# Attention inputs loaded as 48 rows of each half, in two DMAs, with r and v in one buffer

## The reference, cut to what matters

```python
for t in range(S):
    y[:, :, t] = np.einsum('bhd,bhde->bhe', rt, state)
    Sa = np.einsum('bhde,bhe->bhd', state, at)
    state_decay = state * wt[:, :, None, :] - np.einsum('bhd,bhe->bhde', Sa, bt)
    state = state_decay + np.einsum('bhd,bhe->bhde', vt, kt)
```

## Time and profile before

| | |
|---|---|
| Time, median of 3 runs | 1083.21 us (1082.46 to 1086.68) |
| Span of the profiled execution | 1081.6 us (its own device time is not listed; 1.6 us below the median) |
| Busy: TensorE matmul, VectorE, ScalarE, GpSimd | 974.9, 605.9, 316.1, 285.7 us |
| Moved | 159.61 MB in 119,984 packets, mean 148 GB/s |
| `t_in` loads | 48 of 776 KB |
| `rr`, `vt`, `vtm` loads | 24 each of 384, 256 and 240 KB |

### The profile page before, as it was taken

The page is one execution under the profiler, slowest core; times in us unless marked ns, Lnnn a source line. Parts: engine busy times, 40 slices in busy tenths (PEclk is TensorE's granted clock), DMA queues, the critical chain, the costliest instruction groups (busy, mean ns, idle before and its releaser), DMA issues. The chain is left out here.

```text
span 1081.6 us, 47466 instructions
## 1 busy us (share of the span) xinstructions
PE 974.9 (90%) x21177; PEld 853.5 (79%) x21178; DVE 605.9 (56%) x981; ACT 316.1 (29%) x737; POOL 285.7 (26%) x351
## 2 busy tenths in 40 slices
PE   3425879999999998999999999979999999999997
PEld 3425769889888866888878888848999999999997
DVE  8896957898988761111211111146656565655655
ACT  5434645655555500011010010031121222222211
POOL 1008989798910003116611100051101000000000
PEclk9999977999999989999999999999999999999999
DMA  6877656998888537996884544320010101010100
GB/s 230 227 176 213 212 162 196 248 262 254 255 248 260 159 116 252 318 307 216 249 274 160 163 160 162 117 79 25 25 25 25 25 1 25 1 25 2 25 1 25
DMA packets 119984, 159.61 MB, mean 148 GB/s; under 512 B 60164, under 2 KB 91028, under 8 KB 119540
## 3 DMA queue, kind: packets, MB, share of 16 engines
q1 hardware_dynamic: 105636, 125.12, 38.5%
q0 software_dynamic: 5824, 25.28, 7.8%
q10 hardware_dynamic: 8464, 8.43, 2.4%
HBM read 133.15 MB, written 19.23 MB: 141 GB/s over the span
## 5 line engine op out<-in xcount | busy, mean ns | idle before, releaser
L1102 DVE TENSOR_SCALAR ht<-h_bank 128x512 f32<-128x512 f32 x62 | 42.8, 691 | 233.4 <-PE h_bank L1079 233.3
L1365 ACT CAST g_hi<-g 128x512 fp32r<-128x512 f32 x96 | 59.6, 620 | 278.6 <-DVE g L1319 278.6
L1090 PE MATMUL y_bank<-w_all,ht 128*128 x496 | 140.4, 437 | 0.3 <-DVE ht L1102 0.3
L1090 PEld LDWEIGHTS y_bank<-w_all,ht 128*128 128x128 f32 x496 | 92.7, 192 | 35.6 <-issue 1.9
L1234 PE MATMUL y_bank<-w_out_hi,g_hi 128*128 128x320 f32 x380 | 118.0, 311 | 1.4 <-DVE g_lo L1299 1.4
L1079 PE MATMUL h_bank<-xt,w 128*128 128x128 f32 x992 | 119.0, 278 | 0.0
L1234 PE MATMUL y_bank<-w_out_hi,g_lo 128*128 128x320 f32 x380 | 117.5, 309 | 0.0
L1234 PE MATMUL y_bank<-w_out_lo,g_hi 128*128 128x320 f32 x380 | 117.3, 309 | 0.0
L1079 PEld LDWEIGHTS h_bank<-xt,w 128*128 128x128 f32 x992 | 113.1, 192 | 3.8
L1221 PE MATMUL h_bank<-xt_hi,w_in_hi 128*128 128x512 f32 x288 | 113.8, 395 | 0.5 <-DVE xt_hi L1282 0.5
L1221 PE MATMUL h_bank<-xt_hi,w_in_lo 128*128 128x512 f32 x288 | 112.6, 391 | 0.0
(11 more groups left out here) (207 smaller groups left out, 1763.4 us busy)
## 6 DMA issues: line engine op xcount, KB each, us to landing
w<-w_in SPq DMA_DIRECT2D x31, 1024.0 KB, 5.9
t_in<-wab_in SPq DMA_DIRECT2D x24, 776.0 KB, 6.2
t_in<-wak_in SPq DMA_DIRECT2D x24, 776.0 KB, 6.7
w_all<-w_in POOLq DMA_DIRECT2D x8, 1280.0 KB, 8.9
rr<-rr_in SPq DMA_DIRECT2D x24, 384.0 KB, 3.3
w_rest<-w_in SPq DMA_DIRECT2D x62, 128.0 KB, 3.1
vt<-vt_in SPq DMA_DIRECT2D x24, 256.0 KB, 3.9
vtm<-vtm_in SPq DMA_DIRECT2D x24, 240.0 KB, 3.4
```

The lines of the kernel that those rows point to most:

```text
L1090: last = pe.matmul(y_bank[s][:, 0:FEAT], ht[s][:, f, :], w2[:, ds(e * W2 + f * FEAT, FEAT)], start=f == 0, stop=f == NF - 1)
L1102: dve.tensor_scalar(ht[s][:, FH * n:FH * n + FH, :].rearrange("q f t -> q (f t)"), h_bank[s][n][:, :], 0.0, None, ALU.max).then_inc(s_relu, 1)
L1365: act.copy(g_hi[j % RING][:, :], g[j % 2][:, :]).then_inc(s_ghi, 1)
```

## The change

Three things are changed. A `t_in` load is issued as two DMAs, one for each half; from the fourth load on each brings 48 rows of the half in place of 64 (`filled`), and VectorE waits for 32 in place of 16. The first three loads still bring all 64 rows, so that the rows not loaded later hold the padding of an earlier load. `rr` and `vt` become parts of one buffer `vr` with 20 blocks of 64 columns, loaded as 48 rows of each half in two DMAs, where `rr` was loaded and with its wait for `m2`. `load_vt`, with its wait for `m1`, is gone.

```diff
+FILLED = 48
+
+
+def filled(i):
+    return slice(HALF * i, HALF * i + FILLED)
...
-        g2, m1, m2, sat, vt = (m_.sb(n, [PARTS, HS, C]) for n in ("g2", "m1", "m2", "sat", "vt"))
-        rr = m_.sb("rr", [PARTS, HS + HP, C])
+        g2, m1, m2, sat = (m_.sb(n, [PARTS, HS, C]) for n in ("g2", "m1", "m2", "sat"))
+        vr = m_.sb("vr", [PARTS, 2 * HS + HP, C])
+        rr, vt = vr[:, 0:HS + HP, :], vr[:, HS + HP:2 * HS + HP, :]
...
-                sp.dma_start(t_in[j % TR][:, :], src).then_inc(s_t[j % TR], 16)
+                for h in two:
+                    part = rows(h) if j < TR else filled(h)
+                    sp.dma_start(t_in[j % TR][part, :], src[part, :]).then_inc(s_t[j % TR], 16)
...
-            def load_rr(k):
+            def load_vr(k):
                 if k >= 1:
                     sp.wait_ge(did["m2"], k)
-                sp.dma_start(rr[:, :, :], inp["rr"][k]).then_inc(s_vt_rr, 16)
+                for h in two:
+                    sp.dma_start(vr[filled(h), :, :], inp["vr"][k][filled(h)]).then_inc(s_vr, 16)
...
-            def load_vt(k):
-                if k >= 1:
-                    sp.wait_ge(did["m1"], k)
-                sp.dma_start(vt[:, :, :], inp["vt"][k]).then_inc(s_vt_rr, 16)
...
                 if k == 21:
-                    load_rr(0)
+                    load_vr(0)
...
                 if k == STEPS - 2:
                     load_vtm(0)
-                    load_vt(0)
...
                 if more:
                     load_vtm(k + 1)
-                    load_vt(k + 1)
                 if k + 2 < STEPS:
                     load_inverses(k + 2)
                 if more:
-                    load_rr(k + 1)
+                    load_vr(k + 1)
...
-                dve.wait_ge(s_t[j % TR], 16 * (j // TR + 1))
+                dve.wait_ge(s_t[j % TR], 32 * (j // TR + 1))
...
-                arrive(s_vt_rr, 32 * i)
+                arrive(s_vr, 32 * i)
...
-    arrays["vt"] = halves(by_head(v))
-    arrays["rr"] = halves(np.concatenate([by_head(r), other_half(by_head(r))], axis=3))
+    arrays["vr"] = halves(np.concatenate([by_head(r), other_half(by_head(r)), by_head(v)], axis=3))
```

More of the change, by code:

```diff
@@ L234, in attention @@
         s_blk, s_tt = ([[m_.sem(f"{n}{s}_{part}") for part in range(GROUP)] for s in range(3)] for n in ("s_blk", "s_tt"))
-        s_ax_vtm, s_vt_rr = (m_.sem(n) for n in ("s_ax_vtm", "s_vt_rr"))
+        s_ax_vtm, s_vr = (m_.sem(n) for n in ("s_ax_vtm", "s_vr"))
         s_step, s_step_dve = m_.sem("s_step"), m_.sem("s_step_dve")
```

## The result

The change takes 1094.04 us (median of 20 runs, 1084.99 to 1102.83) against 1083.18 us for the kernel before in the same session (20 runs, 1077.10 to 1088.55). The ratio is 1.0093, with a 95% interval of 1.0070 to 1.0115: slower by 0.9%. The forecast was 1078.2 us, with a chance of 0.08 for slower, so it had the wrong sign. The profiled execution of the change took 1094.93 us with a span of 1093.1 us; the span before was 1081.6 us.

What follows compares the result with a forecast made beforehand. Bounds: VectorE's waits for `t_in` behind a late queue in the first stage, TensorE in the second. Savings 2.1 + 1.2 + 0.8 + 1.0 - 0.1 = 5.0 us gave 1078.2 us; forecast's own range 1075 to 1082, overall 1070 to 1084.

Steps and rivals of the forecast that it cites:

- the first of the sum: Bytes of the attention loads: a `t_in` load takes 0.48 us less transfer time, `rr` and `vt` as `vr` 0.40 less.
- Waits at 39 to 48 us, 2.1 us less: First stage: most of VectorE's 2.36 us of waits for `t_in` go; 2.1 us taken, bounds 1.0 to 2.36.
- at 81 and 87 us, 1.2 less: First stage, after the inversion by halves: VectorE's 2.34 us of `t_in` waits shrink by 1.2 us, bounds 0 to 2.34.
- the sign that I had named: First stage: VectorE has no wait for `t_in` from 28 to 52 us if the forecast is right.
- First loads, 0.1 us more: Start of the first stage: three full loads in two DMAs each lengthen the wait by 0.1 us, at most 0.43.
- Standstills of TensorE at 80 to 107 us, 0.8 less: First stage: 8.2 us of standstills, taken for instruction fetches, shorten by 0.8 us; bounds 1.5 worse to 3 better.
- Wait for `ax`, 1.0 less: Start of the second stage: TensorE's 1.18 us wait for `ax` shrinks by 1.0 us, bounds 0 to 1.18.
- Issues, 0: Both attention stages: 48 more `t_in` issues on SP, 0.43 to 0.56 us each, cost nothing, covered by SP's waits.
- `vt` with `rr`, 0: Second stage: loading `v` with `r` after `m2` costs nothing, as `vr` lands some 2 us early.
- the clock stays up: Rival, start of second stage: TensorE avoids the fall to 1.2 GHz, saving about 7.5 us more; 1070.7 us, chance 0.28.
- Late `vr`: Rival, second stage: TensorE waits 1.1 us for `vr` in each of 23 steps, 25 us; 1103 us, chance 0.07.
- The small packets as pace: Rival: small packets pace the queue, `t_in` lands hardly sooner, only 1 us is saved; 1082.2 us, chance 0.20.

Runs made afterwards that it cites:

- the single parts: Against the change: `vr` by halves with `t_in` whole, ratio 0.9972 and 0.9982 to the kernel before; `t_in` by halves with `vr` whole, 1.0052.

## Why the prediction was wrong

**The step that failed** is the first of the sum: "In the stretch in which nothing but such loads runs, the engines move 413 GB/s at a share of 1.00, so a load shrinks from 1.92 to 1.44 us of transfer time, 0.48 us less." The 413 GB/s are the rate of loads that fill all 128 partitions. I carried it over to loads that fill 48 of one half, for which the trace of before had no row, and gave it no bounds. Loads that fill the 64 rows of one half move 224 to 237 GB/s (the expectations above estimate 211 from the first loads). An estimate: at 231, the pair of 0.596 MB needs 2.6 us, 0.7 us more than the whole load, and `vr` with 0.492 MB needs 2.1 us where `rr` and `vt` needed 1.6. A step of the second stage has one of each, 1.2 us of engine time more, in a step whose engines were busy for 0.89 of 9.45 us, or 8.4 us. The sum, 9.6 us, is more than the step has. Measured over the whole execution, the two prices are 0.6 and 0.3 us; from 180 to 300 us, by the shares of the single parts, they are 0.10 and 0.07 of 9.45 us, 1.6 us together, which says the same more strongly. The prediction had every number for this but the rate.

The prediction said that "on how a 48-row DMA is spread the trace has no row", and then took comfort from the rule of the Trainium skill, page "DMA: Bandwidth & Descriptors", section "Why a DMA increments its semaphore by 16 and not by 1", that 48 rows keep all 16 engines. The trace agrees with that rule, as far as it goes: the share is 0.99 from 4 to 8 us, where each DMA has 64 rows, and 1.06 from 180 to 300 us, where most have 48. Busy engines are not fast engines. The rule that speaks against this change stands on another page of the Trainium skill, "SBUF — State Buffer", section "Door 1: The DMA port swizzle (why `[64,N]` ≈ `[32,N]`)": the port that a transfer uses depends on the partition, and partitions 0 to 63 reach 8 of the 16 ports; it gives 196 GB/s for a transfer to these and 328 GB/s for one to all 128, at 1 MiB. This case agrees, with 231 against 413, both above the page's figures. Read for the prediction, it would have been a rival with the right sign.

**Waits at 39 to 48 us, 2.1 us less; at 81 and 87 us, 1.2 less.** Wrong with the first step: 2.82 and 2.95 us are waited for in place of 2.36 and 2.34, and the sign that I had named, no wait of VectorE from 28 to 52 us, didn't come.

**First loads, 0.1 us more.** Mis-sized: 1.82 us. The bound, "one issue, 0.43 us at most", counted the issue and no transfer. The first load keeps its 0.795 MB, and at 231 GB/s that takes 3.4 us instead of 1.9; 1.5 of the 1.8 us are this.

**Standstills of TensorE at 80 to 107 us, 0.8 less.** It is 8.6 us, against 8.2. There was not less engine time of loads in the way, so the term is not tested by the change; that these standstills are fetches is not shown by any run either.

**Wait for `ax`, 1.0 less.** The wait of 1.18 us at the start of the second stage is gone, as the step says. But the stage starts at 147.2 in place of 145.2, so that `ax` only had more time to arrive, and in later steps TensorE waits 1.4 us for it.

**Issues, 0.** The cover that I named, SP's wait for the product that frees `vtm`, holds where SP isn't held: 1.12 us for the pair, and the step is 9.45 us. It doesn't hold against a full queue, which turns the pair into 3.2 to 4.4 us. Even and odd rows, with as many issues, hold SP for at most 2.7 us in the same stretch and lose nothing, so it is the queue and not the issue.

**`vt` with `rr`, 0.** Right. TensorE waits for `vr` once, 0.3 us, and whole or by halves `vr` costs nothing alone.

**The rivals.** That the clock stays up didn't happen: the 3.06 us standstill is there to the hundredth, and the clock is 0.50 from 163 to 177 us. Late `vr` was priced at 25 us for a wait in each step and didn't happen. The small packets as pace are not what made this kernel slower, since even and odd rows change the time and no small transfer. That fewer bytes buy nothing is what this rival said too, though, and rows 0 to 111 fit it. The rival that came true is one I didn't have: the loads themselves get slower.

What stays open: the profiles place 9.2 us of the median's 10.9 in attention in one execution, and in others of the slow versions less (the profiled run with the first three loads whole ended attention 2.1 us after the kernel before, where its median is 10.7 us above). The slow versions also spread more, 20 us with the first loads whole against 13 us for the kernel before in the same session. The granted clock explains little of the change's loss: its mean over the change's runs is 0.986, and at that clock the kernel before lies at 1082 to 1084 us in the other sessions, so that 10 to 12 us remain (an estimate; the clocks of the kernel before in the change's own session are not on record). Why the loss of one version differs so much from execution to execution is not settled.

## What to carry to other kernels

Ask of a load which partitions one DMA fills before you count its bytes: two loads of 48 rows, each in one half, together cost 0.6 us more engine time here than one load of 128 rows with a third more bytes. If a load must be split, split it so that each part still spans both halves. And where a price is carried from one shape to another, give it bounds in both directions, even when it looks like plain bytes over bandwidth; an edit that lowers the bytes can raise the DMA share, and that share in the steady stage, against 1, is a good sign of whether it will be felt (here from 0.99 on, with one small exception at 0.92).

## What the runs showed of the hardware

From 4 to 8 us, DMAs of 64 rows in one half of the partitions moved 224 to 237 GB/s, those of all 128 rows 413 to 421, and those of every other row 315 to 323 GB/s. All kept the engines at 0.88 to 1.03 busy. The rate of every other row is that of a start: over the whole execution these loads cost no more engine time than whole ones (414 and 418 us). Two loads of 48 rows, one in each half, cost 0.6 us more engine time than one of 128 rows.

Two such DMAs at once, on two queues and into different halves, came to 237 GB/s together. The Trainium skill, page "SBUF — State Buffer", section "Can I just issue two DMAs to hit both halves?", answers no, with a gain of 6% measured; the gain here is 3% over the change's 231 GB/s, where the two halves stand behind one another on one queue. Why they don't add up no run here shows.

One DMA of rows 0 to 111 landed no sooner than one of all 128 rows, with an eighth fewer bytes (8.2 and 7.6 us), and the engines were busy with SP's queue for longer (427 and 418 us).

An issue on SP is no fixed price: the pair took 1.12 us with room in the queue and up to 4.36 us without, and what stands behind it on SP is late by as much.
